# Attention steps in twos on TensorE, ScalarE and VectorE, with the next head's rounding one step later

## The reference, cut to what matters

```python
# attention: B, H, S, D = 4, 8, 576, 64, blockwise causal (blocks of 64)
scores = q @ k.T / sqrt(D); scores = where(block_i >= block_j, scores, -1e9)
attn = exp(scores - max); attn = attn / (sum + 1e-9)
x = (attn @ v) -> (2304 tokens, 512)
# first network: 2304 x 512 -> 2048 -> 512
h = x @ w_in; g = maximum(0.01 * h, h); x2 = g @ w_out
# second network: 8 experts of 512 -> 1024 -> 512, the best one for each token
# with x2 @ w_skip > 0; the other tokens pass through
out = x2 + gate * (relu(x2 @ w1[e]) @ w2[e])
```

## Time and profile before

| | |
|---|---|
| median of 3 runs | 786.81 us (786.13 to 787.49) |
| profiled execution | 787.97 us, of which span 786.2 us |
| PE busy | 761.7 us (97%), 4738 matmuls |
| DVE busy | 368.5 us (47%) |
| ACT busy | 301.4 us (38%) |
| POOL busy | 148.8 us (19%) |
| granted clock, mean | 0.998 |
| first split scores on PE (step 52) | 77.48 us |
| end of the products of the last pair | 315.6 us |
| PE's waits between 70 and 316 us, as listed | 8.8 us |

### The profile page before, as it was taken

How to read it: one execution, slowest core, us unless ns; L and a number is a source line. 1 busy time by engine, 2 the same in 40 slices (tenths; PEclk the granted TensorE clock), 3 DMA queues, 4 the chain that set the end, 5 groups by cost and what they waited for, 6 DMA issues and landing times.

```text
span 786.2 us, 13538 instructions
## 1 busy us (share of the span) xinstructions
PE 761.7 (97%) x4738; PEld 643.4 (82%) x4738; DVE 368.5 (47%) x771; ACT 301.4 (38%) x711; POOL 148.8 (19%) x193
## 2 busy tenths in 40 slices
PE   7999989999999998999999999999999999999997
PEld 3555878888888887999987877878778879999996
DVE  5667455543343554013355554555554342444644
ACT  4566655544444554234432222222221131333533
POOL 3226564221121231100020000000000031222222
PEclk9999999999999999999999999999999999999999
DMA  4344767554444541365665656556462038777750
GB/s 125 96 126 142 211 197 201 160 143 130 118 137 128 147 116 57 93 214 162 191 174 177 196 150 190 144 178 189 142 192 68 28 114 246 234 226 236 235 172 4
DMA packets 97671, 121.68 MB, mean 155 GB/s; under 512 B 14226, under 2 KB 60578, under 8 KB 97608
## 3 DMA queue, kind: packets, MB, share of 16 engines
q1 hardware_dynamic: 94776, 116.50, 50.4%
q0 software_dynamic: 2080, 3.77, 1.5%
q10 hardware_dynamic: 752, 0.59, 0.2%
HBM read 89.35 MB, written 31.57 MB: 154 GB/s over the span
## 4 chain that ended last, share of the span: by engine, by line
PE 91%; ACT 2%; issue 2%; SPq 1%; DVE 1%; DMA 1%; POOL 1%; DVEq 0%; POOLq 0%; ACTq 0%
PE ps_hid L1731 10%; PE ps_h L1520 9%; PE ps_x L1573 9%; PE ps_x L1575 8%; PE ps_x L1574 8%; PE ps_h L1522 8%; PE ps_h L1521 8%; PE ps_o L1502 5%; PE ps_t L1476 4%; PE ps_y L1743 3%; PE ps_y L1744 3%; PE ps_y L1742 3%; PE ps_s L1427 2%; PE ps_s L1463 2%; PE ps_s L1464 1%
## 5 line engine op out<-in xcount | busy, mean ns | idle before, releaser
L1520 PE MATMUL ps_h<-xh,win_h 128*128 128x384 f32 x384 | 136.5, 355 | 3.1 <-ACT act L977 2.4
L1522 PE MATMUL ps_h<-xh,win_l 128*128 128x384 f32 x384 | 128.9, 336 | 0.0
L1521 PE MATMUL ps_h<-xl,win_h 128*128 128x384 f32 x384 | 128.8, 335 | 0.0
L1573 PE MATMUL ps_x<-wout_h,g_hi 128*128 128x512 f32 x288 | 117.0, 406 | 0.0
L1575 PE MATMUL ps_x<-wout_h,g_lo 128*128 128x512 f32 x288 | 112.5, 391 | 0.0
L1574 PE MATMUL ps_x<-wout_l,g_hi 128*128 128x512 f32 x288 | 112.2, 390 | 0.0
L977 ACT ACTIVATE act<-ps_h 128x384 f32<-128x384 f32 x96 | 47.1, 491 | 154.9 <-PE ps_h L1522 154.9
L965 ACT ACTIVATE prob<-ps_s,neg_max 128x128 f32<-128x128 f32 (+3 forms) x144 | 78.6, 549 | 28.2 <-DVE neg_max L1126 27.6
L1132 DVE COPY pt<-ps_t 128x384 f32<-128x384 f32 (+4 forms) x113 | 48.4, 436 | 82.4 <-PE ps_t L1476 82.1
L1166 DVE TENSOR_TENSOR g_lo<-g_raw,g_hi 128x512 fp32r<-128x512 f32 x72 | 49.5, 688 | 78.0 <-ACT g_hi L987 77.9
L1126 DVE TENSOR_REDUCE neg_max<-ps_s 128x1 f32<-128x128 f32 (+3 forms) x144 | 71.8, 504 | 30.4 <-PE ps_s L1430 15.3
(11 more groups left out here) (185 smaller groups left out, 1053.0 us busy)
## 6 DMA issues: line engine op xcount, KB each, us to landing
w_sb<-in_w SPq DMA_DIRECT2D x64, 512.0 KB, 5.4
hidden<-act SPq DMA_DIRECT2D x96, 192.0 KB, 2.3
g_raw<-hidden SPq DMA_DIRECT2D x72, 256.0 KB, 4.1
k_raw<-in_k_t SPq DMA_DIRECT2D x40, 144.0 KB, 3.1
x2rows<-x SPq DMA_DIRECT2D x18, 256.0 KB, 2.3
out<-x SPq DMA_DIRECT2D x18, 256.0 KB, 2.6
w_stage<-in_w_in SPq DMA_DIRECT2D x16, 256.0 KB, 3.4
w_stage<-in_w_out SPq DMA_DIRECT2D x16, 256.0 KB, 2.8
```

What stands on the lines that cost most here:

```text
L1520: e.matmul(dst, win_h[:, f, kc, :], xh[slot][:, kc, :], start=kc == 0, stop=False)
L1521: e.matmul(dst, win_h[:, f, kc, :], xl[slot][:, kc, :], start=False, stop=False)
L1522: last = e.matmul(dst, win_l[:, f, kc, :], xh[slot][:, kc, :], start=False, stop=kc == KC - 1)
L1573: e.matmul(dst, hi, wout_h[:, f, :], start=f == 0, stop=False)
```

## The change

PE, ACT and DVE get two loops. Up to step 53 (PE) or 55 (ACT, DVE) they go step by step as before. From step 54 each turn of the loop covers two steps s and s + 1:

- PE: the scores of units s + 2 and s + 3; the first half of the hidden groups of both steps; the transposes of units s - 2 and s - 1; the products with V of both steps; the other groups; the inverse.
- ACT: the copies of the first groups; the exponentials of s + 2 and s + 3 with the turned copies between them (an exponential whose buffer frees a unit later, behind the tail, waits for the next turn and comes first there); the other work of steps s + 2 and s + 3 (`between`); the copies of the other groups.
- DVE: the maxima of s + 2 and s + 3, the turned copies of s - 2 and s - 1, o and inverse copies of s and s + 1, the other work of s + 2 and s + 3.

A hidden group is placed whole on a step. `groups_at` gives the groups of two steps in two halves; a single group goes to the second half. Of a head's rounding `high_q`, `high_k`, `low_k` and `copy_k` move from i = 3 and 7 to i = 4 and 8, `low_q` from i = 5 and 0 to 6 and 1, on all engines and SP. `add_epsilon` goes directly behind the pair's last exponential. SP's and POOL's programs stay step by step.

```diff
--- before.py
+++ after.py
@@ -99,23 +99,27 @@
...
     for g in range(N_ATT_HID):
-        for part in range(2):
-            n = 2 * g + part
-            if g < FC:
-                s = 50 + 34 * n // (2 * FC)
-            elif g < 3 * FC:
-                s = 86 + 34 * (g - FC) // (2 * FC)
-            elif g < TWO_BANKS:
-                s = 122 + 22 * (n - 6 * FC) // (2 * (TWO_BANKS - 3 * FC))
-            else:
-                s = N_UNITS + 5 + g - TWO_BANKS
-            at[s].append((g, part))
+        if g < FC:
+            s = 50 + 34 * g // FC
+        elif g < 3 * FC:
+            s = 86 + 34 * (g - FC) // (2 * FC)
+        elif g < TWO_BANKS:
+            s = 122 + 22 * (g - 3 * FC) // (TWO_BANKS - 3 * FC)
+        else:
+            s = N_UNITS + 5 + g - TWO_BANKS
+        at[s].append(g)
     return at
...
-    return [g for g, part in FILL.get(s, ()) if part]
+    return FILL.get(s, ())
+def groups_at(s):
+    groups = FILL[s] + FILL[s + 1]
+    return groups[:len(groups) // 2], groups[len(groups) // 2:]
...
@@ -682,13 +686,13 @@
...
                         load_head(e, 2 * p + 3)
-                    if i == 3 and ROW_PAIRS <= p + 1 < N_PAIRS:
+                    if i == 4 and ROW_PAIRS <= p + 1 < N_PAIRS:
                         copy_k(2 * p + 2)
...
                         load_head(e, 2 * p + 4)
-                    if i == 7 and ROW_PAIRS <= p + 1 < N_PAIRS:
+                    if i == 8 and ROW_PAIRS <= p + 1 < N_PAIRS:
                         copy_k(2 * p + 3)
...
@@ -823,9 +827,9 @@
...
                 if ROW_PAIRS <= p + 1 < N_PAIRS:
-                    if i == 3:
+                    if i == 4:
                         low_k(2 * p + 2)
-                    if i == 7:
+                    if i == 8:
                         low_k(2 * p + 3)
...
@@ -964,6 +968,8 @@
...
                              accum_out=row_sum[p % 2][:, sum_column(u):sum_column(u) + 1]).then_inc(s_exp, 1)
+                if i == UNITS - 1:
+                    add_epsilon(p)
...
@@ -1009,28 +1015,49 @@
...
             load_v(e, 0)
-            for s in range(STEPS):
+            def between(s):
                 p, i = divmod(s, UNITS)
-                if 3 <= s < N_UNITS + 3 and (s - 3) % UNITS in by_act((s - 3) // UNITS):
-                    copy_turned(s - 3)
-                for g in filled_at(s - 1):
-                    copy_hidden(g)
-                if s < N_UNITS:
-                    exponential(s)
                 if ROW_PAIRS <= p + 1 < N_PAIRS:
-                    if i == 3:
+                    if i == 4:
                         high_q(2 * p + 2)
-                    if i == 7:
+                    if i == 8:
                         high_q(2 * p + 3)
...
                     high_w_in(f)
-                if i == 8 and p < N_PAIRS:
-                    add_epsilon(p)
-            for g in filled_at(STEPS - 1):
-                copy_hidden(g)
+            for s in range(ROW_UNITS + 2):
+                if s >= 3 and s - 3 < ROW_UNITS - 2 and (s - 3) % UNITS in by_act((s - 3) // UNITS):
+                    copy_turned(s - 3)
+                if s <= ROW_UNITS:
+                    for g in filled_at(s - 1):
+                        copy_hidden(g)
+                exponential(s)
+                between(s)
+            def behind_tail(u):
+                return (u - P_RING) % UNITS == TAIL
+            for s in range(ROW_UNITS, STEPS, 2):
+                before, behind = groups_at(s)
+                for g in before:
+                    copy_hidden(g)
+                if s + 1 < N_UNITS and behind_tail(s + 1):
+                    exponential(s + 1)
+                if s + 2 < N_UNITS:
+                    exponential(s + 2)
+                for u in (s - 2, s - 1):
+                    if u < N_UNITS and u % UNITS in by_act(u // UNITS):
+                        copy_turned(u)
+                if s + 3 < N_UNITS and not behind_tail(s + 3):
+                    exponential(s + 3)
+                between(s + 2)
+                between(s + 3)
+                for g in behind:
+                    copy_hidden(g)
...
@@ -1166,30 +1193,50 @@
...
-            scale_q(0)
-            for s in range(STEPS):
+            def between(s):
                 p, i = divmod(s, UNITS)
-                if s < N_UNITS:
-                    maximum(s)
-                if 3 <= s < N_UNITS + 3 and (s - 3) % UNITS not in by_act((s - 3) // UNITS):
-                    copy_turned(s - 3)
                 if i == 4 and p + 1 < ROW_PAIRS:
...
                 if ROW_PAIRS <= p + 1 < N_PAIRS:
-                    if i == 3:
+                    if i == 4:
                         high_k(2 * p + 2)
-                    if i == 5:
+                    if i == 6:
                         low_q(2 * p + 2)
-                    if i == 7:
+                    if i == 8:
                         high_k(2 * p + 3)
-                if i == 0 and ROW_PAIRS <= p < N_PAIRS:
+                if i == 1 and ROW_PAIRS <= p < N_PAIRS:
                     low_q(2 * p + 1)
-                if i == 0 and 1 <= p <= N_PAIRS:
+                if i == (0 if p < ROW_PAIRS else 1) and 1 <= p <= N_PAIRS:
                     invert(p - 1)
-                if i == 2 and 1 <= p <= N_PAIRS:
+            scale_q(0)
+            for s in range(ROW_UNITS + 2):
+                maximum(s)
+                if s >= 3 and s - 3 < ROW_UNITS - 2 and (s - 3) % UNITS not in by_act((s - 3) // UNITS):
+                    copy_turned(s - 3)
+                between(s)
+                p, i = divmod(s, UNITS)
+                if i == 2 and p >= 1:
                     copy_inverse(p - 1)
...
                     copy_o(*o_at(s))
+            for s in range(ROW_UNITS, STEPS, 2):
+                for u in (s + 2, s + 3):
+                    if u < N_UNITS:
+                        maximum(u)
+                for u in (s - 2, s - 1):
+                    if u < N_UNITS and u % UNITS not in by_act(u // UNITS):
+                        copy_turned(u)
+                for u in (s, s + 1):
+                    p, i = divmod(u, UNITS)
+                    part = p_v_at(u)
+                    if part and part[3] == (QT if part[1] else 2):
+                        copy_o(part[0], part[1])
+                    if i == 1 and 1 <= p <= N_PAIRS:
+                        copy_inverse(p - 1)
+                between(s + 2)
+                between(s + 3)
...
@@ -1506,22 +1553,19 @@
...
                 e.wait_ge(s_inv, p + 1)
-                if p < ROW_PAIRS:
-                    e.wait_ge(s_of, 2 * p + 1)
+                e.wait_ge(s_of, 2 * p + 1)
                 e.transpose(ps_o[0:UNITS, B_COLS:B_COLS + P], inv[:, :], ident[:, :]).then_inc(s_invp, 1)
-            def hidden(g, part):
+            def hidden(g):
                 m, f = divmod(g, FC)
...
                 dst = ps_hidden(g)
-                if part == 0:
-                    hidden_waits(g)
-                for kc in range(KC // 2 * part, KC // 2 * (part + 1)):
+                hidden_waits(g)
+                for kc in range(KC):
                     e.matmul(dst, win_h[:, f, kc, :], xh[slot][:, kc, :], start=kc == 0, stop=False)
...
                     last = e.matmul(dst, win_l[:, f, kc, :], xh[slot][:, kc, :], start=False, stop=kc == KC - 1)
-                if part:
-                    last.then_inc(s_h, 1)
+                last.then_inc(s_h, 1)
...
@@ -1538,26 +1582,48 @@
...
-            scores_of_both(0)
-            for s in range(STEPS):
-                if ROW_UNITS <= s + 2 < N_UNITS:
-                    scores(s + 2)
-                if 2 <= s < N_UNITS + 2:
-                    transposes(s - 2)
+            def products_with_v(s):
                 p, i = divmod(s, UNITS)
...
                     p_v(*p_v_at(s))
-                if i == 1 and 1 <= p <= N_PAIRS:
+                if i == 1 and 1 <= p <= ROW_PAIRS - 1:
                     turn_inverse(p - 1)
+            scores_of_both(0)
+            for s in range(ROW_UNITS):
+                if ROW_UNITS <= s + 2:
+                    scores(s + 2)
+                if s >= 2:
+                    transposes(s - 2)
+                products_with_v(s)
+                p, i = divmod(s, UNITS)
                 if i in GROUP_AT:
...
                         scores_of_both(n)
-                for g, part in FILL[s]:
-                    hidden(g, part)
+                for g in FILL[s]:
+                    hidden(g)
+            for s in range(ROW_UNITS, STEPS, 2):
+                for u in (s + 2, s + 3):
+                    if u < N_UNITS:
+                        scores(u)
+                before, behind = groups_at(s)
+                for g in before:
+                    hidden(g)
+                for u in (s - 2, s - 1):
+                    if u < N_UNITS:
+                        transposes(u)
+                products_with_v(s)
+                products_with_v(s + 1)
+                for g in behind:
+                    hidden(g)
```

(7 more changed lines are left out.)

## The result

The changed kernel takes 789.0 us in the median of 12 runs (786.23 to 794.11); the kernel before takes 786.87 beside it (12 runs, 786.13 to 788.4). The ratio is 1.0031, with an interval of 1.0019 to 1.0043: slower by 0.3%. The profiled execution took 789.26 us, of which span 787.5. The forecast was 782.0 and faster. (The profiled execution of the kernel before lies 1.2 above its median and this one 0.3, so the two profiles are 1.3 apart where the medians are 2.1.)

A forecast was written before the change was run, and what follows sets the result against it. PE's own stream was taken to bound the kernel, standing still about 18 us. Terms -2.5 - 2.8 - 2.5 + 2.7 + 0.8 - 1.0 + 0.5 = -4.8 gave 782.0 us against the median 786.8; range 776 to 790.

The forecast's parts named there:

- the term "+2.7": Steps 52 to 65: later rounding and key copies make PE 2.7 us later at step 66, replacing 4.2 of stalls.
- the wait for head 15's keys: Before step 66: head 15's key copy issues about 105.3, lands near 109, and its wait hides ACT's earlier waits.
- "-2.5" for steps 86 to 121: Dense steps, two hidden groups per double step: PE's standstill falls from 7.6 to 5.1 us.
- the inverse's own term: Inverse behind the second groups: precision switches of 0.08 to 0.11 us each, nine times, +0.8.
- ACT's lateness: Dense steps: ACT's second-group copy 0.4 and 0.2 us late at i = 6 and 7, some 0.5 on PE per two pairs.
- -2.8: Steps 66 to 85: bank stalls and exponential waits go, except 0.8 of 3.6 us.
- -2.0: Step 122 to the last products: -2.5 us of stalls gone, +0.5 for o's copy ahead of the inverse at the end.
- the -1.0 for fewer changes between scores and transposes: PE, all stretches: half the changes between scores and transposes go, at some 0.02 us each; bounds 0 and -2.
- the two small terms: All stretches together: the inverse's precision switches, +0.8 us, and fewer changes between scores and transposes, -1.0.
- given back: Dense double steps: ACT late by 0.3 to 0.5 us in all 17, adding 4 to 6; about 786.8, chance 0.18.
- The slower rival: Double steps 58 to 64: ACT's early waits hold hidden copies and SP's stores, 3 us four times; 791, chance 0.20.
- the three signs that I had named as proof against me: ACT's first-pair waits over some 6 us, a new transpose wait each double step, or key copies no longer holding PE.

The follow-up runs named there:

- experiment 4: The change plus 20 unused matmuls of 128 columns on PE ahead of the first split scores; 787.25 us against 786.99 for the kernel before, ratio 1.0004.
- experiment 2: The kernel before, step by step, with only the next heads' rounding and key copies one step later; 790.58 us against 786.99, ratio 1.004.
- Experiment 7: The change with double steps and later rounding only from step 72, and ACT copying the second hidden groups first; 784.16 us against 786.74 for the kernel before.
- experiment 9: Double steps from step 72, ACT's second-group copies first, early split heads' key copies ahead of next-head loads on SP; 782.58 us against 786.52 for the kernel before.
- experiments 3: The change with only SP's key copies back at i = 3 and 7, rounding still one step later; 787.66 us against 786.99 for the kernel before.
- 10: The change with key copies of the first two split pairs ahead of next-head loads on SP; 791.75 us against 786.52 for the kernel before.
- 11: The kernel before with key copies of the first two split pairs ahead of next-head loads on SP; 785.47 us against 786.52 for the kernel before.
- experiment 1: The change with the first split pair's rounding and key copies back on their old steps; 787.38 us against 786.99 for the kernel before, ratio 1.0003.
- experiment 8: The change with the first split pair's rounding unshifted and ACT copying second hidden groups first; 787.9 us against 786.74 for the kernel before, ratio 1.0017.
- 5: The change with double steps and later rounding only from step 72, hidden groups whole before that; 785.04 us against 786.74 for the kernel before, ratio 0.9983.

## Why the prediction was wrong

**The step that failed** is the term "+2.7" for steps 52 to 65. Its first half was right in place and size: the first copy of k issues behind the inverse's store and a load of w_in, at 75.59, and the first split scores start 1.3 us later (forecast 1.0). What I made of it was wrong. I counted that delay as covered by the wait for head 15's keys: late at the start, caught up at the end. But the copy makes a wait of 2.4 us where 0.39 stood (the half group that stood ahead of it before is gone from that step too), and after it the clock is 0.50 for 6.8 us. Step 54 then starts 4.3 us late, of which 3.1 vanish when the wait is filled with useless matmuls (experiment 4). Nor do head 15's keys cover it. Their copy issues at 107.97 in the change and at 104.66 in experiment 4 (forecast 105.3): SP's run of issues ahead of it starts at 93.47 instead of 90.35, so the queue is late when PE is. In the kernel without double steps a late PE does catch up there (experiment 2). The term measured +5.6; less the 2.8 that experiment 4 gives back at step 66, it is +2.8, which is the forecast, and head 15's tail scores start at 108.80 there, where I had the keys at 109.1. So the sum of the waits was right and the price of the clock was missing. The prediction had no term for it, though its window rows had a clock column that always read 1.00.

**A second term was mis-sized**, "-2.5" for steps 86 to 121; it measured -0.5. It was the difference of a standstill got by subtraction (7.6, before) and one got from a model (5.1, after). Read directly, gap by gap as the distance between hidden groups less what the same pieces take where nothing waits (two, three and four transposes 0.14, 0.25 and 0.36), the kernel before stood still for 6.1: 6 x 0.43, 4 x 0.36, 4 x 0.13 and 1.6 at the steps with no group. The changed one stands still for 4.6, less than I had set: twice 0.33 + 0.38 + 0.49 + 0.14 + 0.11 + 0.17 + 0.47 + 0.20, in the order of the gaps from step 88 on. That is -1.5. Two things take most of it back. One shows in the dense stretch of the changed kernel (PE):

```profile
190.84 0.28 PE L1511 MATMUL ps_s<-k,q 68*128 68x128 f32 x1
191.07 0.44 PE L1565 MATMUL ps_h<-xh,win_h 128*128 128x384 f32 x1
191.35 0.34 PE L1566 MATMUL ps_h<-xl,win_h 128*128 128x384 f32 x1
...
227.72 0.40 PE L1511 MATMUL ps_s<-k,q 68*128 68x512 f32 x1
227.96 0.36 PE L1565 MATMUL ps_h<-xh,win_h 128*128 128x384 f32 x1
228.16 0.34 PE L1566 MATMUL ps_h<-xl,win_h 128*128 128x384 f32 x1
```

At 191.07 the group had to wait for the bank, and its second matmul starts 0.28 behind the first; at 227.96 it had not, and it is 0.20. Groups behind scores take 2.19 to 2.23 after such a wait and 2.10 to 2.15 without; I had 2.08 for both. There are 8 of these gaps in four pairs, and they cost 8 x 0.08 = 0.6 that the kernel before doesn't pay apart: its waits end behind transposes, whose price holds that hand-over already. The other is the inverse's own term, about 0.1 four times. -1.5 + 0.6 + 0.4 = -0.5. This sum is worked out from rows and no kernel tried it. ACT's lateness was smaller than forecast and in the wrong place: it is 0.33 in each two pairs (0.5 forecast), all of it at i = 8, where ACT's copy comes late behind its other work:

```profile
196.61 0.34 PE L1511 MATMUL ps_s<-k,q 68*128 68x384 f32 x1
197.26 0.45 PE L1565 MATMUL ps_h<-xh,win_h 128*128 128x384 f32 x1 [0.32 <-ACT act L983]
```

The scores there start at 196.19, so this gap is 1.07 instead of 0.74. Experiment 7 removes it and nothing else of this stretch (111.8 us for the same steps, and 111.7 in experiment 9, which has its order).

**The other steps.** The waits for exponentials are gone, and the stalls of steps 66 to 85 with them: -2.2 against -2.8. Steps 122 to the end with the end's own term: -1.6 against -2.0. Of the -1.0 for fewer changes between scores and transposes nothing can be told apart. The wait for head 15's keys was there, at the scores that start at 111.56, with 1.2 against the 1.18 of before, and head 14's had one too (0.92 before 102.13). The misses add up, in the profiles: 2.9 in the first term, 2.0 in the dense steps, 0.6 and 0.4 in the other two, and 0.2 for the two small terms, which is the 6.1 between -4.8 and +1.3. The clock is a little under half of it.

**The rivals.** Leave out the clock's fall, and the change is at 786 to 787.3: experiment 4 has 787.25, the best runs of the change 786.2. That is "given back", 786.8, though by the gaps' true size and not by ACT's lateness, so the match is luck. The slower rival named ACT at the head of its queue; in the change ACT waits there 2.1 and 2.0 for loads of w_in and 0.5 for POOL, and the one copy that PE waits for there costs it 1.1. So "slower" came by another mechanism than that rival's. None of the three signs that I had named as proof against me (over 6 us of ACT's waits, a new wait at transposes, keys that hold nothing) is what made it wrong; ACT's waits come near the first, with 5.5 in five for w_in and 0.5 for POOL between 70 and 320 us. In experiments 3 and 10 the slower rival's mechanism is real: 2.75 and 4.2.

**What stays open:** what decides whether the clock falls behind a wait (below), how the waits for keys in steps 54 to 65 divide between bytes and the order of issues, and whether head 15's copy is late in the change through the clock alone (experiment 4 filled one wait and moved nothing else).

## What to carry to other kernels

A wait on TensorE has two prices, its length and what the clock does after it: look up the granted clock in each stretch behind a wait that the change makes longer, and give a longer wait a second term with a chance of its own. Here a fall lasted 3.4 or 6.8 us at half clock, so by estimate it costs 1.7 or 3.4 beside the wait, unless a later wait takes it up (experiment 2). Before moving work on a chain that crosses an in-order transfer queue, list everything that stands in the queue between the old place and the new one, and start the reordering where that queue is no longer the one that sets the time: from step 72 the double steps, with ACT's copies first, save 2.9 us (experiments 9 and 11), and begun at step 54 they save nothing (experiment 1). Where a stall is found by subtraction before a change and by a model after it, test the model first on the kernel before.

## What the runs showed of the hardware

A single wait of PE can be followed by a fall of the clock to its 1.2 GHz level. In the profiles the clock fell behind waits of 2.37 (the change), 1.68 and 0.91 (experiment 2), 2.75 (3), 2.05 (7), 2.65 (8), 3.69 and 4.16 (10). It stayed at 1.00 behind waits of 1.87 (9, at 126.60), 1.64 (4, at 108.80), 1.57 (5, at 87.31), 1.50 (8, at 133.85) and 1.29 (1), and behind the same wait of 0.91 in the kernel before. So the length of the wait alone does not decide it. The fall begins in the wait itself (the change, 78.73) or up to 1.1 us behind it (experiment 2, 79.70 behind a wait that ends at 78.59). It lasts 6.8 us in the change and in experiment 8, and 3.4 in experiments 2, 3, 7 and 10. Measured against the filled wait, the one in the change costs 3.1 us at step 54 and 2.8 at step 66. The Trainium skill (TensorE: Matmul & The Clock Gate, under What's actually happening) says that the throttled state is the default and that activity releases it. These traces agree so far as a wait stands ahead of each of these falls, and the filled wait had none.

The runs of one kernel spread with it. Those of the change lie between 786.23 us at a mean clock of 1.0 and 794.11 at 0.991, those of experiment 9 between 780.41 and 783.04 at 0.998 to 1.0. So one profile of a kernel with such a wait is not enough to size it: among the twelve runs of the change, some show hardly any fall.
